# A linear-attention recurrence on one core: the first unit's triangular systems dealt over two partitions each, with new issue orders for all engines

## The reference, cut to what matters

```python
for t in range(S):                       # S = 768, batch 4, 8 heads, D = 40
    y[:, :, t] = einsum('bhd,bhde->bhe', r_t, state)
    Sa = einsum('bhde,bhe->bhd', state, a_t)
    state = state * w_t[:, :, None, :] - einsum('bhd,bhe->bhde', Sa, b_t)
    state = state + einsum('bhd,bhe->bhde', v_t, k_t)
x = y.transpose(0, 2, 1, 3).reshape(3072, 320)
h = x @ w_in                             # 320 -> 2048
g = where(h >= 1, h, where(h <= -1, 0, (h + 1) ** 2 / 4))
x = g @ w_out                            # 2048 -> 320
h = maximum(maximum(x @ w1, x @ w2), x @ w3)     # 320 -> 768
return h @ w_last
```

## Time and profile before

| what | value |
|---|---|
| median of 3 runs | 1055.07 us (1054.64 to 1055.91) |
| the profiled execution | 1052.78 us, span 1051.1 us |
| mean granted TensorE clock | 0.97 |
| PE, DVE, ACT, POOL busy | 92%, 48%, 37%, 43% of the span |

### The profile page before, as it was taken

The page is one execution under the profiler, slowest core; times in us unless marked ns, Lnnn a source line. Parts: engine busy times, 40 slices in busy tenths (PEclk is TensorE's granted clock), DMA queues, the critical chain, the costliest instruction groups (busy, mean ns, idle before and its releaser), DMA issues.

```text
span 1051.1 us, 29793 instructions
## 1 busy us (share of the span) xinstructions
PE 962.9 (92%) x12330; PEld 807.1 (77%) x12330; DVE 506.8 (48%) x700; ACT 393.1 (37%) x719; POOL 456.5 (43%) x633
## 2 busy tenths in 40 slices
PE   6648999899998887899999999999999999999998
PEld 5436787788776776677888788878887888888887
DVE  8886666667552452696333323332333243324321
ACT  1214455455554563464233323332333133313321
POOL 3586786959688841242133213321332133123311
PEclk9957999999998899999999999999999999999999
DMA  5854667676645631462000100010001000100000
GB/s 84 142 108 89 119 104 133 102 139 107 128 81 116 116 72 28 135 181 68 1 26 1 31 1 26 0 30 0 25 0 30 0 25 0 30 0 26 0 1 26
DMA packets 242915, 61.27 MB, mean 58 GB/s; under 512 B 223728, under 2 KB 238832, under 8 KB 242800
## 3 DMA queue, kind: packets, MB, share of 16 engines
q1 hardware_dynamic: 147760, 44.86, 19.3%
q10 hardware_dynamic: 95040, 14.76, 8.6%
HBM read 44.89 MB, written 14.68 MB: 57 GB/s over the span
## 4 chain that ended last, share of the span: by engine, by line
issue 27%; PE 17%; POOL 10%; DVE 3%; ACT 1%; DMA 1%; POOLq 0%; DVEq 0%; ACTq 0%; SPq 0%
POOL hid_lo L1399 10%; PE ring L1212 8%; PE acc L1212 5%; PE ring L1222 3%; PE ring L1254 2%; DVE sq L1457 1%; PE acc L1276 1%; DVE clip L1451 1%; DMA raw<-in_moe_w_dram 1%; DVE wmax_lo L1425 1%; ACT sq L1361 0%; ACT hid_hi L1337 0%; POOLq L35 0%; DVE win_lo L1425 0%; DVE wout_lo L1417 0%
## 5 line engine op out<-in xcount | busy, mean ns | idle before, releaser
L1399 POOL TENSOR_TENSOR hid_lo<-sq,hid_hi 128x512 fp32r<-128x512 f32 x132 | 174.4, 1321 | 453.5 <-ACT hid_hi L1337 453.5
L1451 DVE TENSOR_SCALAR clip<-ring 128x512 f32<-128x512 f32 x96 | 66.2, 690 | 132.1 <-PE ring L1222 132.1
L448 POOL TENSOR_TENSOR prod<-sysX 128x30 f32<-128x30 f32 (+14 forms) x193 | 101.8, 527 | 58.1 <-DMA sysX<-systems 42.8
L1337 ACT CAST hid_hi<-sq 128x512 fp32r<-128x512 f32 x132 | 82.0, 622 | 93.5 <-DVE sq L1457 71.5
L1361 ACT ACTIVATE sq<-clip 128x512 f32<-128x512 f32 x96 | 60.7, 633 | 147.7 <-DVE clip L1451 145.9
L452 POOL TENSOR_TENSOR sysX<-sysX,prod 128x30 f32<-128x30 f32 (+14 forms) x193 | 106.9, 554 | 15.1
L1457 DVE SCALAR_TENSOR_TENSOR sq<-clip,sq 128x512 f32<-128x512 f32 x96 | 67.9, 708 | 59.9 <-ACT sq L1361 59.9
L1212 PE MATMUL acc<-hid_hi,wout_hi 128*128 128x512 f32 x192 | 76.4, 398 | 7.7 <-POOL hid_lo L1399 7.6
L1482 DVE TENSOR_TENSOR sq<-ring,clip 128x512 f32<-128x512 f32 x36 | 24.9, 692 | 120.4 <-PE ring L1222 98.1
L1383 ACT COPY clip<-ring 128x512 f32<-128x512 f32 x36 | 21.1, 587 | 153.8 <-PE ring L1222 153.8
L1212 PE MATMUL ring<-x_hi,win_hi 128*128 128x512 f32 x192 | 75.5, 393 | 3.4 <-PEq L958 3.4
(11 more groups left out here) (166 smaller groups left out, 2177.4 us busy)
## 6 DMA issues: line engine op xcount, KB each, us to landing
nat_k<-in_k_dram ACTq DMA_DIRECT2D x48, 80.0 KB, 3.4
vz<-in_v_dram SPq DMA_DIRECT2D x96, 40.0 KB
nat_r<-in_r_dram SPq DMA_DIRECT2D x96, 40.0 KB, 2.8
xT<-yT SPq DMA_DIRECT2D x96, 40.0 KB
out_dram<-res SPq DMA_DIRECT2D x24, 160.0 KB, 1.8
inverses_T<-sysX SPq DMA_DIRECT2D x7, 512.0 KB, 4.5
nat_w<-in_w_dram ACTq DMA_DIRECT2D x44, 80.0 KB
nat_a<-in_a_dram ACTq DMA_DIRECT2D x44, 80.0 KB, 3.5
```

The costliest lines, as they stand in the source:

```text
L448: g_.tensor_tensor(some, X[:, 0:j, j:j + 1].to_broadcast([P, j, rest]), X[:, j:j + 1, j + 1:BLK].to_broadcast([P, j, rest]), ALU.mult)\
L1337: nc.scalar.copy(hid[(u if u < T1 else u - T1) % HB][0][:, :], src).then_inc(hid_hi, 1)
L1399: nc.gpsimd.tensor_tensor(hid[at % HB][1][:, :], sq[at % 2][:, :], f32(hid[at % HB][0][:, :]), ALU.subtract)\
L1451: nc.vector.tensor_scalar(clip[f % 2][:, :], ring[(f + 2) % 4][:, :], -1.0, None, ALU.max).then_inc(clipped, 1)
```

## The change

1. Unit 0 uses all 128 partitions. `sysX[0]` is loaded twice with the full 64 systems, to partitions 0 to 63 and 64 to 127, as the copy from which pivots are read. The running sums go to a second tensor, `row_pairs` (16 rows of 32, lying in `yT`): partitions 0 to 63 hold the even rows of each system, 64 to 127 the odd ones. A step works on (j + 1) // 2 rows in place of j, which makes 2,600 numbers over the 30 steps for each of its two instructions. The load is four DMAs in place of two, of which the two to `row_pairs` (and the two stores of the result, in place of one) move rows of 32 numbers, 128 bytes each. The diagonal is two memsets. `sysX[0]` needs no zeros any more. The semaphore counts are adapted, and in DRAM unit 0 lies as `dram[0, 0, 2 * q + i, j]`.
2. All three order tables, the PSUM assignment, `SOLVE_FROM`, `SOLVE_AT` and `VECTOR_STEPS` (17 to 16) are new. Where the lines below are cut, the tables of ACT and SP for the start and the finish, and the old tables of DVE and POOL for the finish are left out.

```diff
@@ -104,50 +104,51 @@
         loaded = {n: [sem(f"loaded_{n}{i}") for i in range(NATS[n])] for n in names}
 
         ORDER = {
-            "PE": [("g", 0), ("p", 0), ("gs", 0), ("qt", 0), ("dn", 9), ("z", 0), ("ys", 0), ("w", 10), ("yt", 0),
-                   ("vz", 0), ("k", 1), ("a", 9), ("r", 2), ("rr", 0), ("b", 9), ("ak", 1), ("st", -1), ("n", 9),
+            "PE": [("p", 0), ("g", 0), ("a", 9), ("qt", 0), ("gs", 0), ("k", 1), ("b", 9), ("z", 0), ("ys", 0),
+                   ("dn", 10), ("vz", 0), ("n", 9), ("yt", 0), ("st", -1), ("rr", 0), ("w", 11), ("r", 2), ("ak", 1),
                    ("xy", 0)],
-            "ACT": [("load w1", 10), ("load b0", 10), ("load b1", 9), ("load k0", 2), ("rates", 0), ("load k1", 2),
-                    ("p", 0), ("gs", 0), ("qt", 0), ("inverse", 0), ("z", 0), ("w", 10), ("vz", 0), ("r", 2),
-                    ("load w0", 11), ("k", 1), ("load a0", 10), ("b", 9), ("load a1", 11), ("st", -1), ("dense", -1)],
-            "DVE": [("ak", 0), ("inverse", 0), ("x", -1), ("scan", 9), ("y", -1), ("bk", 0), ("dn", 9), ("a", 9),
-                    ("bn", 9), ("dense", -1), ("rr", 0), ("n", 9)],
-            "POOL": [("step", 0), ("step", 0), ("step", 0), ("step", 0), ("step", 0), ("stTc", -1), ("step", 0),
-                     ("step", 0), ("total", -1), ("step", 0), ("step", 0), ("kn", 2)],
-            "SP": [("load v0", 1), ("load r1", 2), ("solved", 1), ("system", 8), ("load r0", 2), ("unit", 8),
-                   ("y", -1), ("inverse", 1), ("load v1", 2), ("dense", -1)],
+            "ACT": [("load a1", 10), ("load k1", 3), ("rates", 1), ("p", 0), ("load b0", 11), ("qt", 0),
+                    ("load a0", 11), ("gs", 0), ("k", 1), ("z", 0), ("b", 9), ("inverse", 0), ("load k0", 3),
+                    ("vz", 0), ("dense", 0), ("st", -1), ("load b1", 11), ("load w0", 13), ("w", 11),
+                    ("load w1", 13), ("r", 2)],
+            "DVE": [("inverse", 0), ("ak", 0), ("bn", 9), ("x", -1), ("y", -1), ("a", 9), ("scan", 10), ("bk", 2),
+                    ("dense", 0), ("dn", 10), ("n", 9), ("rr", 0)],
+            "POOL": [("kn", 1), ("step", 0), ("step", 0), ("step", 0), ("step", 0), ("step", 0), ("stTc", -1),
+                     ("step", 0), ("step", 0), ("total", -1), ("step", 0)],
+            "SP": [("load v0", 1), ("load r1", 2), ("unit", 8), ("dense", -1), ("solved", 1), ("load v1", 2),
+                   ("y", -1), ("inverse", 1), ("load r0", 3), ("system", 9)],
         }
         FINISH = {
-            "PE": [("p", 0), ("a", 5), ("b", 2), ("g", 0), ("qt", 0), ("gs", 0), ("n", 2), ("z", 0), ("r", 0),
-                   ("dn", 6), ("k", 1), ("vz", 0), ("w", 0), ("ys", 0), ("yt", 0), ("rr", 0), ("ak", 1), ("xy", 0),
-                   ("st", 5)],
...
+            "PE": [("a", 9), ("g", 0), ("n", 9), ("r", -1), ("vz", -1), ("p", 0), ("dn", 3), ("w", 12), ("k", 1),
+                   ("rr", -1), ("ys", -1), ("gs", 0), ("yt", -1), ("qt", 0), ("xy", -1), ("b", -1), ("ak", 1),
+                   ("z", 0), ("st", -1)],
...
+            "DVE": [("scan", -1), ("ak", 0), ("a", 13), ("bk", 1), ("bn", 3), ("dense", 10), ("inverse", 0),
+                    ("rr", -1), ("n", 12), ("x", -1), ("dn", -1), ("y", -1)],
+            "POOL": [("step", 0), ("step", 0), ("step", 0), ("step", 0), ("step", 0), ("step", 0), ("step", 0),
+                     ("kn", 2), ("stTc", 6), ("step", 0), ("step", 0), ("total", 10), ("step", 0), ("step", 0)],
...
         }
         START = {
-            "PE": [("n", 7), ("a", 5), ("w", 4), ("r", 15), ("dn", 5), ("k", 19), ("ak", 19), ("b", 6)],
...
-            "DVE": [("step", 0), ("a", 1), ("scan", 0), ("step", 0), ("dn", 1), ("n", 2), ("bn", 1)],
-            "POOL": [("kn", 9), ("step", 0), ("step", 0), ("step", 0), ("step", 0)],
...
+            "PE": [("b", 6), ("ak", 18), ("k", 16), ("w", 3), ("n", 6), ("r", 14), ("a", 4), ("dn", 4)],
...
+            "DVE": [("scan", 0), ("step", 0), ("dn", 1), ("step", 0), ("n", 2), ("a", 0), ("bn", 1)],
+            "POOL": [("step", 0), ("step", 0), ("step", 0)],
...
         }
         START_LEN, FINISH_FROM = 20, 21
-        VECTOR_STEPS, VECTOR_FROM = 17, 10
-        FIRST_STEP = {0: 0, 1: 203}
-        SOLVE_FROM, SOLVE_AT = [3, 3, 5, 4, 4, 4, 8], 0
+        VECTOR_STEPS, VECTOR_FROM = 16, 10
+        FIRST_STEP = {0: 0, 1: 959}
+        SOLVE_FROM, SOLVE_AT = [3, 3, 6, 5, 6, 9, 7], 8
         OPENS = {"gs": "g", "xy": "ys"}
         MORE = {"yt": "ys"}
         READERS = {"xy": ("x", "y")}
-        BANK = {"g": 1, "p": 4, "qt": 4, "dn": 0, "z": 1, "ys": 2, "w": 4, "vz": 1, "k": 0, "a": 3, "r": 4, "rr": 1,
-                "b": 4, "ak": 0, "st": 3, "n": 1}
+        BANK = {"p": 3, "g": 0, "a": 1, "qt": 3, "k": 2, "b": 4, "z": 1, "ys": 2, "dn": 3, "vz": 1, "n": 0, "st": 4,
+                "rr": 1, "w": 4, "r": 3, "ak": 0}
         bank_of = {n: (pair + single)[at] for n, at in BANK.items()}
         OUTS = {"qt": 2, "z": 2}
 
@@ -169,7 +170,7 @@
 
         CONSTS, MASKED, PADDED = 4, 4, 2 + NATS["w"] + NATS["a"] + len(pair + single)
         CLEARED = EARLY + LATE + NATS["r"] + NATS["v"] + 1
-        ZEROED = len(invT) + len(stT) + len(st) + 2
+        ZEROED = len(invT) + len(stT) + len(st) + 1
         SOLVE = 2 * (BLK - 2)
 
         def wanted(n, g):
@@ -208,7 +209,7 @@
             return up_to(u, lambda many: 16 * 4 * many)
 
         def loaded_systems(u):
-            return up_to(u, lambda many: 16 * (1 if many == UNIT else 2))
+            return up_to(u, lambda many: 16 * (1 if many == UNIT else 2)) + (32 if u >= 0 and u % 2 == 0 else 0)
 
         def program(eng, steps):
             for n, at in sequence(eng):
@@ -285,6 +286,21 @@
         def part(x, at, n):
             return x[:, :, :].rearrange("r j (p q d) -> r j p q d", p=HP, q=2)[:, :, :, at, 0:n]
 
+        sums_of_rows = yT[:, :, :, :].rearrange("r j p t -> r (j p t)")
+        row_pairs = sums_of_rows.rearrange("r (m t) -> r m t", t=BLK)
+
+        def place(dram, u, q, i, j):
+
+            return dram[0, 0, 2 * q + i, j] if u == 0 else dram[u % 2, q, i, j]
+
+        def stores(u):
+
+            return 0 if u < 0 else u // 2 + (2 if u % 2 == 0 else 1)
+
+        def diagonals(u):
+
+            return u // 2 + (2 if u % 2 == 0 else 1)
+
         block = ctx.enter_context(nc.Block())
 
         @block.sync
@@ -303,7 +319,7 @@
                     for q in range(2):
                         at = slice(j * CH + q * BLK, j * CH + (q + 1) * BLK)
                         src = nT[g % EARLY][at, :, :, q * BLK:(q + 1) * BLK]
-                        sp.dma_start(sysd[u % 2, q, i, j].rearrange("h m t -> m h t"),
+                        sp.dma_start(place(sysd, u, q, i, j).rearrange("h m t -> m h t"),
                                      src.rearrange("m s p t -> m (s p) t"))\
                             .then_inc(sys_stored[u % 2], 16)
 
@@ -313,10 +329,13 @@
                 if g < first + many - 1:
                     return
                 sp.wait_ge(sys_stored[u % 2], stored_systems(u))
-                ge(sp, x_stored[u % 2], 16 * (u // 2))
+                ge(sp, x_stored[u % 2], 16 * stores(u - 2))
                 if u == 0:
-                    sp.wait_ge(zeroed, ZEROED)
-                if many == UNIT:
+                    src = sysd[0, 0].rearrange("i j h m t -> (i j h) m t")
+                    for odd in range(2):
+                        sp.dma_start(sysX[0][rows(odd), :, :], src).then_inc(sys_loaded[0], 16)
+                        sp.dma_start(row_pairs[rows(odd), :, :], src[:, odd:BLK:2, :]).then_inc(sys_loaded[0], 16)
+                elif many == UNIT:
                     sp.dma_start(sysX[u % 2][:, :, :].rearrange("r m t -> r (m t)"),
                                  sysd[u % 2].rearrange("q i j h m t -> (q i j h) (m t)"))\
                         .then_inc(sys_loaded[u % 2], 16)
@@ -330,9 +349,14 @@
                 u = unit_of[g]
                 if g > UNITS[u][0]:
                     return
-                sp.wait_ge(diag_set[u % 2], u // 2 + 1)
+                sp.wait_ge(diag_set[u % 2], diagonals(u))
                 if u > 1:
                     ge(sp, inverted, UNITS[u - 1][0])
+                if u == 0:
+                    for odd in range(2):
+                        dst = xtd[0, 0].rearrange("i j h m t -> (i j h) m t")[:, odd:BLK:2, :]
+                        sp.dma_start(dst, row_pairs[rows(odd), :, :]).then_inc(x_stored[0], 16)
+                    return
                 sp.dma_start(xtd[u % 2].rearrange("q i j h m t -> (q i j h) (m t)"),
                              sysX[u % 2][:, :, :].rearrange("r m t -> r (m t)")).then_inc(x_stored[u % 2], 16)
 
@@ -341,7 +365,7 @@
                 i = g - UNITS[u][0]
                 if g < 3:
                     sp.wait_ge(zeroed, ZEROED)
-                sp.wait_ge(x_stored[u % 2], 16 * (u // 2 + 1))
+                sp.wait_ge(x_stored[u % 2], 16 * stores(u))
                 ge(sp, done["z"], g - 2)
```

(22 more changed lines are left out.)

8 lines of the change are left out of this document (3 added, 5 removed), and 12 rows, old and new, of tables (FINISH, START).

## The result

The changed kernel is slower. Its median was 1066.03 us (1061.04 to 1073.37) against 1054.64 for the kernel before on the same chip, ratio 1.0135 [1.0105, 1.0164]; measured again beside the last experiments it was 1071.94, ratio 1.0172 [1.0146, 1.0198]. The profiled execution took 1072.92 us, span 1071.2, 20.1 us more than the one before; my sum for it was 1048.4.

A forecast was written before the change was run, and what follows sets the result against it. Only the first 425 us could change, the kn and bk chain bounding most of groups 1 to 14: + 0.5 - 2.3 - 2.6 - 4.0 + 4.0 = -4.4 us, so 1048.4 profiled, 1050 median; forecast 1043 to 1054 (0.45), range 1038 to 1060.

The forecast's parts named there:

- group 0 begins: Group 0's products would begin about 79.7 us, when DVE's steps end, in place of 81.8.
- nine iterations by the chain: Nine iterations of groups 1 to 14, bound by the wait for kn, would average 14.8 us, 133.2 together.
- s = 5, 9, 13: Iterations where a unit ends and few or small steps follow stTc: the chain does not bind, 13.3 us each.
- groups 15 to 20: Groups without scan or reciprocal, bound by POOL's steps or PE's chain: 77.3 us against 79.9, 2.6 less.
- groups 21 to the dense blocks: The new FINISH order fills waits in groups 21 to 23 and the change to dense blocks: 4 us less, between 0 and 7.
- clock, a term of its own: Work lost to lower clock phases where the chain is on top: 4 us, between 0 and 12.
- Rival (b): Slower: PE's wait ahead of each xy lowers the clock in groups 1 to 14; 1055, or 1060; chance 0.20.
- The chain over `kn` and `bk`: From one xy to the next through stTc, three steps, kn, bk, reciprocal and masks: 14.5 to 15.4 us; PE waits about 1.5.
- Rival (a): The kn and bk chain does not bind since POOL reaches kn sooner: 13 us off, 1037; chance 0.19.
- The start: Before group 0: inverses at DVE about 77 us, DVE's steps done at 79.7; gain gone by iteration 0's end, + 0.5.
- Unit 0's solve: POOL's thirty split steps with 2,600 numbers: 25.3 us, 28.8 with collisions, where the trace has 38.5.
- Its loads: Unit 0's two more small-packet DMAs would cost 2 us more, between 1 and 4.

The follow-up runs named there:

- e5: Changed kernel with each later unit's steps on POOL beginning a table later, behind kn: 1069.8 us, ratio 1.0164 to the kernel before.
- e9: Changed kernel with units beginning behind kn and a ninth step place on POOL, ahead of stTc: 1064.8 us, ratio 1.0115 to the kernel before.
- e6: Changed kernel with SP's load of the inverses right behind the store of the solved unit: 1076.78 us, ratio 1.0220 to the kernel before.
- e7: Changed kernel with the inverses' load right behind the solved unit's store on SP, and bk ahead 1: 1062.3 us, ratio 1.0093 to the kernel before.
- e1: Changed kernel with bk ahead 1 in place of 2 on DVE: 1051.16 us, ratio 0.9964 to the kernel before.
- e10: Changed kernel with bk ahead 1, nine step places on POOL, and units beginning behind kn: 1048.23 us, ratio 0.9950 to the kernel before.
- e2: Kernel before with only the split of unit 0, keeping its old tables, banks and step counts: 1050.55 us, ratio 0.9968 to the kernel before.
- e14: Changed kernel with bk ahead 1, nine places, units beginning behind kn, and SP's inverse load ahead of y's store: 1055.82 us, ratio 1.0003.

## Why the prediction was wrong, by its own steps

| step | forecast, us | measured, us | off by |
|---|---|---|---|
| group 0 begins | 79.7 | 81.12 | + 1.4 |
| group 0 | 20.1 | 21.58 | + 1.5 |
| s = 1 and 14 | 29.3 | 26.94 | - 2.4 |
| nine iterations by the chain | 133.2 | 137.53 | + 4.3 |
| s = 5, 9, 13 | 39.9 | 54.04 | + 14.1 |
| groups 15 to 20 | 77.3 | 85.25 | + 8.0 |
| groups 21 to the dense blocks | 36.9 | 38.05 | + 1.1 |
| clock, a term of its own | 4.0 | in the rows above | - 4.0 |

The rows add up to 24.0 of the 24.5 us by which the profiled execution missed its sum.

**The step that failed** is "It does not bind where a unit ends and the steps after `stTc` are few or small: s = 5, 9, 13 (13.3 each)". That few steps stand there is right. But the first of them waits for the unit's load, 5.45 us at s = 9 and 7.12 at s = 13, with `kn` behind it, and at s = 5 the inverses are 4.23 us late. I had put both waits at nothing. The wait for the load comes from the place of the unit's first step ahead of `kn`: without it `bk` no longer waits there, and s = 13 took 16.03 us in place of 19.70 (e5). The time did not fall, since inverses came late elsewhere, 4.11 us at s = 9. Why they are late is only in part known. The eight places make a unit longer, 55 to 58 us against 44 to 47, and I had read the diff's lost place as a shorter list, not as a longer unit. But with nine places they were no sooner there (e9): the solved units then waited in SP's list, where `solved` had moved behind `unit`, which I had not looked at. What that costs stays open.

**The groups after them** are the same step at second hand. Seven of the nine chain iterations came out at 14.38 to 15.36 us, where 14.5 to 15.4 was forecast; s = 6 and 7, behind the late inverses, took 16.91 and 17.02 at clocks of 0.72 and 0.90. Groups 15 to 20 had late inverses twice (2.11 us at 332.59, 4.21 at 346.89), and 17 us at the lower level. I had summed them at full clock; at 0.90 these groups are like those before (0.91), whose loss I should have left in.

**The clock** was set at 4 us between 0 and 12. By windows the lower level has 24 us of groups 1 to 14 and 17 of groups 15 to 20; half of that is work lost, 20.5 us, part of it hidden by waits, against 10 us in the same groups before. Group 0 has another 14 us at the lower level, where it had 9. Rival (b) had the right sign, and its mechanism in part. The clock fell behind the long stalls at the ends of units, but at s = 7 it fell ahead of `xy`, behind two short waits of PE (1.39 us for the reciprocal at 206.21, 0.44 for the mask), and `xy` took 3.63 us in place of 1.97:

```profile
207.97 3.63 PE L708 MATMUL pair<-vz,kb 128*64 128x128 f32 x32 [0.44 <-DVE vz L904]
208.00:210.00 2.00, 2.00 (x20) 2.00 (x22) 1.24 (x3) 0.99 (x2) 1.55 (x3) 0.52 0.65 105
```

At s = 2, 3, 4, 8, 10, 11 and 12, which have such waits too, it stayed at 1.00.

**The chain over `kn` and `bk`** was right in place, releaser and length. Rival (a) priced its absence at 13 us; measured, it is 13 to 18 (e6 with e7, e1, e9 with e10). That e1 ends at 1051 and not at 1037 goes with late inverses (22.5 us of DVE's waits) and the clock (27 us at the lower level in groups 1 to 14), which rival (a), built on my sum, did not have either.

**The start** was right within 1.5 us. DVE's steps ended at 79.60, forecast 79.7; 1.0 of the 1.4 us in the table is the product `p`, which the new list puts ahead of the one that I count from. Unit 0's solve took 30.4 us, forecast 28.8 (where the sum takes 0.0036 us per number, not the 0.0037 written beside it, a matter of 0.2 us). Its loads cost more than I took, 9.2 us from first issue to first use (30.44 to 39.68) where the two plain ones had taken 4.4: 4.8 more, over the upper bound of 4. What I missed is that the plain loads double too, 256 KB each in place of 128, since each half of the partitions gets all 64 systems. In the list of DMAs from 28 to 42 us the median time to landing (last column) tells the two kinds apart:

```profile
yT<-systems SPq DMA_DIRECT2D x2, 128.0 KB, 5.9
sysX<-systems SPq DMA_DIRECT2D x2, 256.0 KB, 4.8
```

Here the Trainium skill's rule on transfers below 512 bytes ("DMA: Bandwidth & Descriptors", Specifications) fits the loads: 128 KB in rows of 128 bytes landed 1.1 us later than twice as much in whole rows. Each small load was issued right behind a plain one, and no run separates the two. The small stores cost nothing more: they landed in 2.9 us (median), and the one plain store before in 2.8 (73.80 to 76.62). The loads did not move group 0 either, since DVE's steps ended only at 79.60 and the inverses were there by 79.63.

**The best version** by its median is e10: the changed kernel with `bk` ahead 1, nine places, and units that begin behind `kn`, 0.5% faster than before; e1 and e2 cannot be told from it. What stays open: how much of its late inverses `solved` ahead of `unit` would cure, since the three tries through SP's list (e6, e7, e14) moved `inverse` alone and made it slower; and why one place is worth 14 us in the old orders, 7 with `bk` ahead 2 (where the start of the units moved as well) and nothing clear with `bk` ahead 1.

## What to carry to other kernels

Count the places that a background job has per period against the work of a whole job with the DMAs at both its ends, not only against the iteration. Then look at the queue that issues these DMAs: a job that is ready sooner gains nothing if its store stands behind another wait. When a table puts a consumer ahead of its producer, list what stands behind the consumer: such a wait cost 18 us in one order, and in another, where it was longer and the clock fell more, 88. And if an iteration is priced without stalls, look at what the first instruction of the next job waits for, and whether something urgent is queued behind it.

## What the runs showed of the hardware

The clock fell where PE had been idle and came back while it was busy. Around the late inverses of s = 5, some windows of 2 us of the changed kernel:

```profile
174.00:176.00 2.00, 0.93 (x18) 0.68 (x14) 0.00 (x0) 1.00 (x2) 0.44 (x2) 1.00 0.97 158
176.00:178.00 2.00, 0.73 (x29) 0.74 (x31) 1.24 (x3) 0.00 (x0) 0.00 (x0) 0.84 0.54 82
178.00:180.00 2.00, 2.00 (x48) 1.82 (x42) 1.18 (x3) 0.37 (x1) 1.26 (x3) 0.50 0.36 56
184.00:186.00 2.00, 2.00 (x51) 1.79 (x51) 0.66 (x2) 0.72 (x2) 1.92 (x3) 0.50 0.40 80
188.00:190.00 2.00, 2.00 (x65) 1.60 (x67) 1.97 (x2) 1.04 (x2) 1.76 (x4) 1.00 0.23 34
```

PE is busy for 0.93 and 0.73 us of the two windows before the fall, then wholly busy at 0.50, the lower level of 1.2 GHz, until about 187, and at full clock from there. So a stall of 2.3 us on PE (at 177.26) was followed by some 10 us at half speed, some 5 us of work, which is more than the stall. Runs of one kernel differ by this too: two profiles of the changed kernel had 24 and 17 us at the lower level in groups 1 to 14, with the same long iterations.
